# Low parts of a Strassen product moved from GpSimd to VectorE, with new places and another order for its combined weights

## What is computed

```python
# attention (decayed, no softmax), 4 x 8 heads x 576 tokens x 64
ret = (q @ k.T / 8) * Dmat
x = (ret @ v) -> 2304 tokens x 512
# first layer, d_ff = 1536
xn = x / sqrt(mean(x * x) + 1e-6) * rms_g
x = (silu(xn @ w_gate) * (xn @ w_val)) @ w_out
# second layer, d_ff = 2048
h = x @ w_in
g = where(h >= 1, h, where(h <= -1, 0, (h + 1) ** 2 / 4))
out = g @ w_out2
```

## Time and profile before

| what | before |
|---|---|
| device time, median of 3 runs | 897.19 us (897.04 to 899.83) |
| the profiled execution | 897.38 us, span 895.6 us |
| TensorE busy (matmul) | 856.9 us, 96% of the span |
| VectorE busy | 648.3 us, 72% |
| ScalarE busy | 490.9 us, 55% |
| GpSimd busy | 240.1 us, 27%, none of it after 526 us |
| granted TensorE clock, mean | 0.99 of full speed |

### The profile page before, as it was taken

How to read it: one execution, slowest core, us unless ns; L and a number is a source line. 1 busy time by engine, 2 the same in 40 slices (tenths; PEclk the granted TensorE clock), 3 DMA queues, 4 the chain that set the end, 5 groups by cost and what they waited for, 6 DMA issues and landing times.

```text
span 895.6 us, 17847 instructions
## 1 busy us (share of the span) xinstructions
PE 856.9 (96%) x7332; PEld 833.9 (93%) x7332; DVE 648.3 (72%) x856; ACT 490.9 (55%) x736; POOL 240.1 (27%) x134
## 2 busy tenths in 40 slices
PE   8999999999999999579999868999999999999998
PEld 5888999999999999579999868999999989999998
DVE  5698866678856447939646697758586988978884
ACT  4667644447554644345334548878687855433331
POOL 1335354446764444462232740000000000000000
PEclk9999999999999999899999989999999999999999
DMA  9991322323335337141440102352425673444442
GB/s 256 259 274 47 109 83 95 100 96 107 97 99 171 101 105 243 55 146 32 140 159 1 48 1 93 114 177 107 153 106 194 224 248 113 130 136 119 140 118 71
DMA packets 109008, 113.46 MB, mean 127 GB/s; under 512 B 6784, under 2 KB 85696, under 8 KB 108928
## 3 DMA queue, kind: packets, MB, share of 16 engines
q1 hardware_dynamic: 108928, 112.33, 40.1%
HBM read 74.55 MB, written 37.75 MB: 125 GB/s over the span
## 4 chain that ended last, share of the span: by engine, by line
PE 86%; POOL 3%; DVE 3%; issue 3%; DMA 1%; SPq 1%; ACT 1%; POOLq 0%; DVEq 0%; ACTq 0%
PE pair L795 16%; PE pair L797 16%; PE pair L796 16%; PE pair L997 5%; PE pair L996 5%; PE pair L995 5%; PE pair L885 4%; PE pair L887 4%; PE pair L886 4%; PE pair L739 2%; PE pair L966 2%; PE pair L967 2%; PE pair L965 2%; PE pair L750 2%; PE pair L687 1%
## 5 line engine op out<-in xcount | busy, mean ns | idle before, releaser
L795 PE MATMUL pair<-xc,wc 128*128 128x288 f32 x672 | 199.5, 297 | 0.2
L796 PE MATMUL pair<-xc,wc 128*128 128x288 f32 x672 | 198.2, 295 | 0.0
L797 PE MATMUL pair<-xc,wc 128*128 128x288 f32 x672 | 197.6, 294 | 0.0
L1138 ACT ACTIVATE cp<-pair 128x576 f32<-128x576 f32 x160 | 103.4, 646 | 153.2 <-PE pair L797 148.3
L1995 POOL TENSOR_TENSOR wc<-wt,wc 128x512 fp32r<-128x512 f32 x78 | 115.5, 1505 | 124.9 <-ACT wc L1064 100.4
L795 PE MATMUL pair<-xc,wr 128*128 128x288 f32 x448 | 134.5, 300 | 13.1 <-ACT cp L1138 7.6
L796 PE MATMUL pair<-xc,wr 128*128 128x288 f32 x448 | 133.4, 298 | 0.0
L797 PE MATMUL pair<-xc,wr 128*128 128x288 f32 x448 | 132.9, 297 | 0.0
L795 PEld LDWEIGHTS pair<-xc,wc 128*128 128x128 f32 x672 | 125.9, 187 | 1.1 <-issue 0.9
L797 PEld LDWEIGHTS pair<-xc,wc 128*128 128x128 f32 x672 | 126.6, 188 | 0.0
L796 PEld LDWEIGHTS pair<-xc,wc 128*128 128x128 f32 x672 | 126.2, 188 | 0.0
(11 more groups left out here) (157 smaller groups left out, 1774.5 us busy)
## 6 DMA issues: line engine op xcount, KB each, us to landing
b_scratch<-cb SPq DMA_DIRECT2D x32, 576.0 KB, 2.9
a_scratch<-cb SPq DMA_DIRECT2D x24, 576.0 KB, 2.9
y<-a_scratch SPq DMA_DIRECT2D x16, 864.0 KB, 6.6
wt<-wB SPq DMA_DIRECT2D x72, 128.0 KB, 2.8
bt<-b_scratch SPq DMA_DIRECT2D x28, 256.0 KB, 2.8
bt<-b_scratch SPq DMA_DIRECT2D x56, 128.0 KB, 3.0
a_k<-kT SPq DMA_DIRECT2D x16, 288.0 KB, 5.7
a_q<-qT SPq DMA_DIRECT2D x16, 288.0 KB, 5.0
```

The source lines that it names most:

```text
L795: pe.matmul(o, wh, xh, start=FIRST[i] and j == 0, stop=False, skip_group_check=True)
L796: pe.matmul(o, wh, xl, start=False, stop=False, skip_group_check=True)
L797: mm = pe.matmul(o, wl, xh, start=False, stop=j == 1, skip_group_check=True)
L1138: act.activation(copied(g, n)[:, :, :], pair[(X, Q, X, X)[n]][:, :, 0:HALF], ACT.Copy).then_inc(s_c, 1)
```

## The change

- All low parts of the second product, of its weights (`wo_lo`) and of its inputs (`y_lo`), and all low parts of unit 12 and of tiles 4 and 5 go to VectorE. GpSimd's queue ends after the first layer's weights (unit 11). `s_wolp` and `s_wold` become one counter `s_wol`, `s_ylp` and `s_yld` become `s_yl`, which counts in the order of the products.
- `wo_at` gives A11, S1 and S2 other places. S1's raw values now take the place of A21's (`wo_raw`), and A11 is loaded in step 16, beside A21 and A22, where it was loaded in step 22.
- The sums and the high and low parts of the combined weights are made at other points: before, one sum in step 17, two in step 22, one behind step 23, and most high parts from step 22 on; now two sums in step 17, one in step 18, one in step 23, with the high parts of A22, A11, S3, S2 in steps 17 to 20 and the low parts of A22, A11, S3 in steps 18 to 20.
- T2's low part no longer waits for T4's sum. SP reloads y11 first, behind T2's low part and T4's sum, where it reloaded y22 first. Unit 12's load waits for one product fewer of the last tile.

The core of the diff:

```diff
-Y_BY_POOL = (B22, T4)
-Y_BY_DVE = (B11, T1, B21, T2, T3)
-WO_SUMS = (S1, S3, S2, S4)
-WO_HIGH = (A22, S1, A11, S2, A12, S3, S4)
-WO_BY_POOL = (A22, A11, S1, S3, S2, S4)
+WO_SUMS = (S3, S1, S2, S4)
+WO_HIGH = (A22, A11, S3, S2, S1, A12, S4)
+WO_LOW = (A22, A11, S3, S1, A12, S2, S4)
...
-        wo_at = (z_w, z_wo11 + WO, z_w + WO, z_wo11, z_w + 2 * WO, z_wo11 + 2 * WO, z_wo6)
+        wo_at = (z_wo11, z_w, z_w + WO, z_wo11 + WO, z_w + 2 * WO, z_wo11 + 2 * WO, z_wo6)
...
                     sp.wait_ge(s_xld, 4 * NT)
+                    load_wo(A11, 0)
                     load_wo(A21, 2)
                     load_wo(A22, 3)
                 if g == GB - 2:
 
                     sp.wait_ge(s_p, 7 * (GB - 2))
-                    load_wo(A11, 0)
                     load_wo(A12, 1)
...
-                sp.wait_ge(s_ylp, 2 * t - 1)
+                sp.wait_ge(s_yl, 7 * (t - 1) + T2 + 1)
+                sp.wait_ge(s_yT, 4 * t)
+                load_y(t, 0, 0)
+
+                sp.wait_ge(s_yl, 7 * (t - 1) + B22 + 1)
                 load_y(t, 1, 1)
...
-            sp.wait_ge(s_yp, 7 * (NT - 1) + A12 + 1)
-            sp.wait_ge(s_ylp, 2 * NT - 1)
+            sp.wait_ge(s_yp, 7 * (NT - 1) + S1 + 1)
+            sp.wait_ge(s_yl, 7 * (NT - 1) + B22 + 1)
             load_unit(2 * UB)
...
                 if g == 2 * UB + 5:
+                    wo_sum(S3)
                     wo_sum(S1)
-                if g == GB - 2:
-                    wo_sum(S3)
+                if g == 2 * UB + 6:
+                    wo_lo(A22)
                     wo_sum(S2)
+                if g == 2 * UB + 7:
+                    wo_lo(A11)
+                if g == 2 * UB + 8:
+                    wo_lo(S3)
                 if g == GB - 1:
+                    wo_lo(S1)
                     y_lo(0, B11)
+                    wo_sum(S4)
                     y_sum(0, T1)
...
             y_lo(0, T1)
             gated(GB - 1)
-            wo_sum(S4)
-            wo_lo()
+            wo_lo(A12)
...
                 else:
+                    unit_sums(2 * UB)
                     tile_sums(NT)
+                    for i in (A11, S1, A12, S2):
+                        unit_lo(2 * UB, i)
+                        token_lo(NT, i)
                     y_c11(t)
-                    for i in (T1, T2):
-                        tile_lo(NT, i)
                     y_c12(t)
-                    for i in (T3, T4):
-                        tile_lo(NT, i)
+                    for i in (S4, S3, A22):
+                        unit_lo(2 * UB, i)
+                        token_lo(NT, i)
                 y_c22(t)
                 y_c21(t)
             tile_sums(NT + 1)
-            for i in T_BY_DVE:
-                tile_lo(NT + 1, i)
+            for i in range(7):
+                token_lo(NT + 1, i)
             tile_sums(NT + 2)
...
             unit(2 * UB - 1)
-            for i in WO_BY_POOL:
-                wo_lo(i)
-            for t in range(NT):
-                for i in Y_BY_POOL:
-                    y_lo(t, i)
-            unit(2 * UB)
-            tile(NT)
-            tile(NT + 1)
```

More of the change, by code:

```diff
@@ L372, in copied, with wo_raw @@
             return (copies if g < GB else copies2)[n]
+        def wo_raw(i):
+            return wo21[:, :, :] if i in (S1, A21) else wot[i][:, 1, :, :]
         def y_slot(t, i):
@@ L1160, in wo_hi @@
                     act.wait_ge(s_woS, WO_SUMS.index(i) + 1)
-                act.activation(wo[i][:, 0, :, :], wot[i][:, 1, :, :], ACT.Copy).then_inc(s_woh, 1)
+                if i == S1:
+                    act.wait_ge(s_p, 7 * (GB - 2))
+                act.activation(wo[i][:, 0, :, :], wo_raw(i), ACT.Copy).then_inc(s_woh, 1)
             def y_hi(t, i):
@@ L1233, in _ @@
                     tile_hi(g - 2 * UB + 3, T3)
+                if g == 2 * UB + 5:
+                    wo_hi(A22)
                 if g == 2 * UB + 6:
-                    wo_hi(A22)
+                    wo_hi(A11)
+                if g == 2 * UB + 7:
+                    wo_hi(S3)
+                if g == 2 * UB + 8:
+                    wo_hi(S2)
                 if g == GB - 1:
                     y_hi(0, B11)
-                    wo_hi(S2)
                 copy(g, 3)
@@ L1244, in _ @@
                 fresh_weights(g, 2)
-                if g == 2 * UB + 6:
+                if g == GB - 2:
                     wo_hi(S1)
-                if g == GB - 2:
-                    wo_hi(A11)
+                    wo_hi(A12)
                 if g == GB - 1:
                     y_hi(0, T1)
-                    wo_hi(A12)
             silu(GB - 1)
-            wo_hi(S3)
             y_hi(0, B21)
+            wo_hi(S4)
             for t in range(NT):
                 y_hi(t, T2)
-                if t == 0:
-                    wo_hi(S4)
                 y_copy(t, 0)
@@ L1724, in wo_sum, with wo_lo @@
                     dve.wait_ge(d_wo[1], 16)
-                    dve.wait_ge(s_p, 7 * GB)
-                    dve.tensor_tensor(wot[S4][:, 1, :, :], wot[A12][:, 1, :, :], wot[S2][:, 1, :, :],
-                                      ALU.subtract).then_inc(s_woS, 1)
-            def wo_lo():
-                dve.wait_ge(s_woh, WO_HIGH.index(A12) + 1)
-                dve.wait_ge(s_woS, 4)
-                dve.tensor_tensor(wo[A12][:, 1, :, :], wot[A12][:, 1, :, :], wo[A12][:, 0, :, :].bitcast(F32),
-                                  ALU.subtract).then_inc(s_wold, 1)
+                    dve.wait_ge(s_p, 7 * (GB - 1) + 2)
+                    dve.tensor_tensor(wo_raw(S4), wo_raw(A12), wo_raw(S2), ALU.subtract).then_inc(s_woS, 1)
+            def wo_lo(i):
+                dve.wait_ge(s_woh, WO_HIGH.index(i) + 1)
+                dve.wait_ge(s_woS, {A22: 2, A11: 3, S3: 3, S1: 3}.get(i, 4))
+                dve.tensor_tensor(wo[i][:, 1, :, :], wo_raw(i), wo[i][:, 0, :, :].bitcast(F32),
+                                  ALU.subtract).then_inc(s_wol, 1)
             def y_sum(t, s):
@@ L1836, in _ @@
                     y_sum(0, T2)
-                y_sum(t, T4)
-                y_lo(t, T2)
+                    wo_lo(S2)
+                    y_lo(t, T2)
+                    y_sum(t, T4)
+                    wo_lo(S4)
+                    y_lo(t, B22)
+                else:
+                    y_lo(t, T2)
+                    y_sum(t, T4)
+                    y_lo(t, B22)
                 y_lo(t, T3)
-                if t == NT - 1:
-                    unit_sums(2 * UB)
                 if t < NT - 1:
                     y_c11(t)
+                y_lo(t, T4)
+                if t < NT - 1:
                     y_lo(t + 1, B11)
@@ L2002, in tile_lo @@
                                    xc[T][:, i, 0, :, :].bitcast(F32), ALU.subtract).then_inc(s_xlp, 1)
-            def wo_lo(i):
-                pool.wait_ge(s_woh, WO_HIGH.index(i) + 1)
-                pool.wait_ge(s_woS, {A22: 1, A11: 3, S1: 3, S3: 3, S2: 4, S4: 4}[i])
-                pool.tensor_tensor(wo[i][:, 1, :, :], wot[i][:, 1, :, :], wo[i][:, 0, :, :].bitcast(F32),
-                                   ALU.subtract).then_inc(s_wolp, 1)
-            def y_lo(t, i):
-                x = yp[y_slot(t, i)]
-                pool.wait_ge(s_yh, 7 * t + i + 1)
-                if i == B22:
-                    pool.wait_ge(s_yT, 4 * t + 2)
-                pool.tensor_tensor(x[:, 1, :, :], y_raw(t, i), x[:, 0, :, :].bitcast(F32), ALU.subtract).then_inc(s_ylp, 1)
             def unit(un):
```

59 lines of the change are left out of this document (22 added, 37 removed).

## The result

The changed kernel takes 877.70 us (median of 4 runs, 877.23 to 878.15), the kernel before 897.71 us in the same session (4 runs, 897.04 to 899.83): a ratio of 0.977, interval 0.9755 to 0.9791. The forecast was 876.5 us. The profiled execution took 877.77 us, span 876.0.

The account below looks back on a forecast made before the run. TensorE, busy 96% of the span, was taken as the bound, with time only in its waits and reduced clock. Gains accumulating to 21.9 us, less a 1.05 us cost: 897.38 - 21.9 + 1.05 = 876.5 us, range 873 to 880 (chance 0.62).

Parts of the forecast that it names:

- Turns: VectorE and GpSimd instructions that both read SBUF operands run one at a time, alternating; GpSimd's turn in step 18 about 1.25 us.
- Part 1: Start of the second product: without GpSimd's low parts the fifth product starts 10.7 us sooner; gain 12.2 us by its end.
- the fourth wait: Start of the second product: TensorE waits 2.7 us before the fourth product, which starts at 376.8.
- Part 2: The second product's four tiles: VectorE's 23.5 us per tile stays hidden beside TensorE's 33.6; gain so far 13.7 us.
- its 1.5 us: Second product behind the fifth product: 1.5 us over 23 x 4.8, put down to the same turns, goes away.
- Part 3: Start of the second layer: unit 12's load lands earlier, VectorE works without a stop, tile 6's first sum moves by 21.9 us.
- Part 4: Steps 17 to 20: GpSimd still makes weights' low parts, so turns come back; cost 1.05 us, from step 18.
- an engine that kept the port while its queue is full: Case in steps 17 to 20: if VectorE keeps its place, the cost is nothing and the sum 875.5 us.
- the first rival of the list: The second layer's start stays as slow, VectorE's instructions being long for another reason than GpSimd: 886 to 888 us; chance 0.13.
- The clock did fall: Rival: the clock falls in a new wait, costing 1.4 to 3.0 us: 878 to 882 us; chance 0.07.
- the granted clock stays at 1.00 in both places: Sign: no clock drop at the start of the second product or at the start of the second layer.
- GpSimd's busy time was to fall to about 155 us: Sign: handing over its low parts cuts GpSimd's busy time from 240 to about 155 us.

Follow-up runs that it names:

- start_back: Changed kernel with the second layer's start as before: GpSimd again makes low parts of unit 12 and B11, B21, B22 of tiles 4 and 5; 883.15 us.
- start_only: Kernel before with one part changed: VectorE alone makes the low parts of unit 12 and of tiles 4 and 5; 893.81 us, ratio 0.996.
- y_back: Changed kernel with the low parts of B22 and T4 of the four tiles on GpSimd again; 883.53 us.
- wo_back: Changed kernel with all seven low parts of the combined weights on GpSimd, in the changed order; 881.95 us.
- extra_tt: Changed kernel plus useless GpSimd work behind step 23: one clear, then 12 subtractions of a 128x576 tile from itself; 888.71 us.
- extra_set: Changed kernel plus 25 useless GpSimd memsets of a 128x576 tile behind step 23; 880.84 us.
- a22_late: Changed kernel with A22's low part made by VectorE in step 22 instead of step 18; 876.07 us.
- after_again: Changed kernel run once more, unchanged, as a yardstick; 879.00 us.
- load_late: Changed kernel with unit 12's load one product later again; 881.92 us.
- start2: Changed kernel with A22's low part in step 22, VectorE's step 23 reordered, and copies and joins moved earlier at the second layer's start; 872.49 us.
- start3: Kernel of start2 with copies (26,1), (26,2), (27,1) ahead of parabolas and joins of steps 24 to 26 earlier; 867.38 us, ratio to kernel before 0.9656.

## Why the prediction was right

The median lies 1.2 us above the forecast. The profiled execution is 1.27 above, and 1.0 of that is attention (76.72 against 75.72).

- **Turns.** Right. The five kernels that put SBUF-reading work back on GpSimd or took it off (start_back, start_only, y_back, wo_back, extra_tt) all moved the way they say, and extra_tt with extra_set shows that it is GpSimd's reading that holds VectorE. The size of a turn was over-estimated for the extra work (0.95 for 1.3 us) and slightly in step 18 (1.10 and 1.09 for 1.25).
- **Part 1.** After taking 2.05 us off (attention's 1.00, part 4's 1.05), the products start at 357.3, 364.5, 376.9 and 382.3; predicted were 357.3, 364.5, 376.8, 382.3. The fifth starts 8.73 us sooner by the record, 10.8 by this count (10.7 predicted). One row was off: the fourth wait, 2.7 predicted, is 1.00 here, because the clock fell behind the second wait and a slower product filled the gap. Where the fall came behind the fourth wait instead, in a22_late and after_again, the rest is 0.6 and 0.8 us longer.
- **Part 2.** Right. PE is busy for 100.00 us between 400 and 500, VectorE for 77.87 of them: covered. The second product ends at 499.6, 497.5 after the 2.05. The cause given for its 1.5 us is only in part right: behind the fifth product the kernel before has one wait, 0.93 us at 424.55, beside VectorE low parts in GpSimd's turns; most of the rest is the fifth product's half clock, which lasted from 393.06 to about 396.5 and cost 1.7 us, not 1.4.
- **Part 3.** Right. T4's low part was due 482.0 - 1.96 + 2.05 = 482.1 and starts at 482.34; tile 6's first sum was due 508.55 and starts at 508.71. PE's first wait is 2.27 (2.2 predicted). load_late shows that this chain has no slack and that the load, 1.3 us ahead of T4's low part (1.1 by the prediction: 480.9 and 482.0), does not set it.
- **Part 4.** Right to 0.03 us: 1.05 predicted, 1.02 to 1.05 by a22_late; an engine that kept the port while its queue is full would have cost nothing here. Its rows in the kernel after, VectorE's queue in step 18, then PE's wait:

```profile
302.66 2.85 DVE L1714 TENSOR_TENSOR wot<-wo,wot 128x1536 f32<-128x1536 f32 x1
305.43 1.84 DVE L1692 TENSOR_TENSOR cb<-cp,cp 128x576 f32<-128x576 f32 x1
...
308.07 0.40 PE L794 MATMUL pair<-xc,wc 128*128 128x288 f32 x1 [0.73 <-ACT cp L1130]
```

  One wait there was not foreseen: c11 of step 17 waited 4.17 us for the store of step 15, probably since A11's load now stands ahead of that store in SP's queue (no run moves the load back). In this profile it stayed inside the step's slack. In the profiles of start_back, load_late and start2 the same join waited 5.8 to 5.9 us and c12 of step 18 came 1.4 to 1.5 us later; in both kernels without that load in step 16 (before, start_only) it did not. So the change has a cost of up to 1.5 us in some executions that the prediction put at nothing, and it was luck that the profiled one was spared.
- **The rivals.** The second layer's start did not stay slow: all its VectorE instructions last 0.68 to 0.76 us, so handing work to VectorE, though it was the busier of the two there, made the stage shorter. (This is the first rival of the list; the prediction's text calls it the second.) By the Trainium skill's page "Perfetto Trace Analysis" (Optimizing Scalar/DVE Operations) offloading may help where VectorE is saturated, though perhaps not to GpSimd; start_back does that offloading and is 5.3 us slower. The clock did fall, which the prediction gave 0.07 and priced at 1.4 to 3 us; against the sum no cost is to be seen, since the waits behind took it up: the fourth product's shrank from 2.7 to 1.00, the one at 511.43 from 3.0 to 1.57. That was luck of place: in after_again, where the first fall came behind the fourth product's wait and no long wait of the second product followed, the rest is 0.8 us longer.
- **Named wrong:** "the granted clock stays at 1.00 in both places". The stretches say otherwise (0.69 and 0.50), and the clock column of the page's 40 slices is too coarse to show it:

```profile
368.00:372.00 4.00, 4.00 (x23) 4.00 (x23) 4.00 (x3) 0.29 (x1) 0.00 (x0) 0.69 0.39 147
...
508.00:510.00 2.00, 1.86 (x8) 1.51 (x7) 1.97 (x4) 0.51 (x1) 0.00 (x0) 0.50 0.00 0
```

Named as a sign and off in size: GpSimd's busy time was to fall to about 155 us and fell to 163.6; the prediction counted what GpSimd hands over and not that GpSimd's own low parts get longer (115.5 to 124.0 us). PE did not wait for them.

What stays open: the three parts put back cost 5.3, 5.8 and 6.3 us, 17.4 in sum, of the 20.6 that the whole gives, and the later load of unit 12 alone costs 3.6. These do not add up to the whole by right: y_back contains a late load as well, and each holds up to 0.8 us of clock. How much of the gain the new order of sums and places gives by itself was not measured.

## What to carry to other kernels

Where VectorE's instructions are longer than their size gives, look at what GpSimd reads at that time: when both engines read two SBUF operands, as all of GpSimd's low parts here do, they take turns, so sharing such work between them does not add their speeds, and the faster one alone can be quicker even where it is the busier. What fits beside it: VectorE's joins with one operand in PSUM kept their 0.74 to 0.75 us beside GpSimd, and GpSimd's clears cost VectorE nothing. (Whether such a join delays GpSimd was not looked at.) Ask too what a slower engine's low parts release: in y_back it was a load, which started 5.0 us late. And after each wait that is removed, ask for the next instruction in the same queue that waits for somebody else: start2 took every wait out of two steps and lost nearly all of it to one copy behind one parabola; start3 showed that the queue's order, not its load, was the cause: it has the same instructions in another order.
